# Gate logits of five chunks in four column quarters, and the gather of token rows moved ahead of the old output rows

## What is computed

```python
logits = x @ w_gate
noise_scale = np.log1p(np.exp(x @ w_noise))
noisy_logits = logits + noise_scale * noise
top2 = np.argpartition(-noisy_logits, 2, axis=1)[:, :2]
...
h = np.maximum(x[mask] @ w1[e], 0.0)
out[mask] += top2_w[mask, k, None] * (h @ w2[e])
```

## Time and profile before

| | us |
|---|---|
| median of 3 runs | 1023.05 |
| lowest, highest | 1022.73, 1024.32 |
| the profiled execution | 1022.97 |
| its span, first to last instruction | 1021.1 |

### The profile page before, as it was taken

How to read it: one execution, slowest core, us unless ns; L and a number is a source line. 1 busy time by engine, 2 the same in 40 slices (tenths; PEclk the granted TensorE clock), 3 DMA queues, 4 the chain that set the end, 5 groups by cost and what they waited for, 6 DMA issues and landing times.

```text
span 1021.1 us, 22022 instructions
## 1 busy us (share of the span) xinstructions
PE 1005.7 (98%) x5982; PEld 871.4 (85%) x5983; DVE 396.3 (39%) x784; ACT 430.6 (42%) x736; POOL 208.3 (20%) x198
## 2 busy tenths in 40 slices
PE   9999999999999999999999999999998999999996
PEld 7889999999999999999888888888887888888885
DVE  3565632432532423425553222242366354222221
ACT  3337754544555455557532222242354453222221
POOL 4540000020010200200332222222322232322222
PEclk9999999999999999999999999999999999999999
DMA  8753450000000000052316222243277342211111
GB/s 272 253 170 125 147 190 1 1 32 0 0 31 0 0 31 0 10 207 90 117 33 223 68 62 64 66 137 132 88 243 256 121 156 73 82 52 52 52 48 45
DMA packets 47078, 95.27 MB, mean 93 GB/s; under 512 B 19245, under 2 KB 24749, under 8 KB 42928
## 3 DMA queue, kind: packets, MB, share of 16 engines
q1 hardware_dynamic: 24240, 66.26, 19.2%
q0 software_dynamic: 10992, 27.84, 8.6%
q10 hardware_dynamic: 11808, 0.68, 0.8%
HBM read 78.98 MB, written 20.37 MB: 97 GB/s over the span
## 4 chain that ended last, share of the span: by engine, by line
PE 92%; DMA 3%; issue 2%; POOL 1%; ACTq 1%; DVE 0%; ACT 0%; SPq 0%; DVEq 0%; POOLq 0%
PE bank L701 27%; PE bank L703 26%; PE bank L702 26%; PE bank L833 3%; PE bank L780 2%; PE bank L652 2%; PE bank L626 2%; PE bank L756 1%; DMA xg<-x_rows,meta_x 1%; PE bank L645 1%; PE bank L612 1%; PE bank L665 1%; DMA out<-ysb,meta_y 1%; PE bank L750 1%; DMA lists<-rec,slot 0%
## 5 line engine op out<-in xcount | busy, mean ns | idle before, releaser
L701 PE MATMUL bank<-ew,hT_hi 128*128 (+1 forms) x328 | 131.9, 402 | 2.6 <-DVE hT_lo L1432 2.6
L701 PE MATMUL bank<-ew,xgT_hi 128*128 (+1 forms) x328 | 131.9, 402 | 0.7 <-issue 0.7
L701 PE MATMUL bank<-xs_hi,mw 128*128 (+1 forms) x384 | 130.0, 338 | 0.0
L703 PE MATMUL bank<-xs_hi,mw 128*128 (+1 forms) x384 | 129.6, 337 | 0.0
L702 PE MATMUL bank<-xs_lo,mw 128*128 (+1 forms) x384 | 129.0, 336 | 0.0
L703 PE MATMUL bank<-ew,xgT_lo 128*128 (+1 forms) x328 | 128.5, 392 | 0.0
L703 PE MATMUL bank<-ew,hT_lo 128*128 (+1 forms) x328 | 128.4, 391 | 0.0
L702 PE MATMUL bank<-ew,hT_hi 128*128 (+1 forms) x328 | 127.8, 390 | 0.0
L702 PE MATMUL bank<-ew,xgT_hi 128*128 (+1 forms) x328 | 127.6, 389 | 0.0
L520 POOL DMA_INDIRECT lists<-rec,slot x36 | 35.8, 994 | 389.5 <-DVE slot L1336 380.3
L701 PE MATMUL bank<-mw,g_hi 128*128 128x512 f32 x288 | 115.1, 399 | 0.0
(11 more groups left out here) (185 smaller groups left out, 1664.1 us busy)
## 6 DMA issues: line engine op xcount, KB each, us to landing
raw<-w_ex SPq DMA_DIRECT2D x32, 1024.0 KB
stage<-w_ff SPq DMA_DIRECT2D x16, 512.0 KB, 3.4
out<-blank SPq DMA_DIRECT2D x3, 1536.0 KB, 11.4
x_rows<-x2sb SPq DMA_DIRECT2D x6, 768.0 KB, 3.9
kbuf<-kN SPq DMA_DIRECT2D x16, 256.0 KB, 3.2
vbuf<-vN SPq DMA_DIRECT2D x16, 256.0 KB, 4.7
qbuf<-qT SPq DMA_DIRECT2D x15, 256.0 KB, 3.9
xg<-x_rows,meta_x POOLq DMA_INDIRECT x43
```

Source lines behind the costliest of these rows:

```text
L701: pe.matmul(o, a_hi, b_hi, start=first, stop=False)
L703: return pe.matmul(o, a_lo, b_hi, start=False, stop=last)
```

## The change

The gate of the five chunks: the three tiles' transposes come at steps 2, 3 and 4 of PE, and ACT copies them at the head of its steps 4, 5 and 6 into one transposed buffer of 384 tokens, for which the memory of `xs_hi` (for the last of the five, of `xs_lo`) is used, since that chunk's input is no longer needed. At step 5, four products with `wg` as the stationary operand (32 columns, 16 of them zeros) and 384 moving columns are formed, each block k of the width in column quarter k of the array, and so in partitions 32k to 32k+31 of bank 7. ACT copies the bank to `lgT` at the head of its step 7. At step 6, PE forms for each tile one product with `lgT` as the stationary operand and a matrix of zeros and ones (in `small`) that adds up the four quarters and turns the logits back. One copy by DVE at step 8 takes all 48 columns. PE's loop over four chunks becomes a loop of two passes with two chunks each. In the last chunk, steps below 10 use the ordinary activation buffer.

The experts: in POOL's step, the gather of tile g+3 comes ahead of the old rows of tile g. In ACT's step, the list of tile g+4 is asked for first, after a wait for the gather of tile g+2, which read the same buffer of `meta_x`.

```diff
+    small[:, 8:24] = i[:, None] % 32 == np.arange(16)
...
+        x2T_in, _ = place("x2T_in", [P, 2, KT, TOK], F32, R_T)
+        x2T_late, _ = place("x2T_late", [P, KT, TOK], F32, R_T + 2 * KT * TOK * 4)
...
-        x2T, R_C = place("x2T", [P, KT, P], F32, a)
+        lgT, R_C = place("lgT", [P, 512], F32, a)
...
-        wg, a = place("wg", [P, KT, 16], F32, a)
+        wg, a = place("wg", [P, KT, 32], F32, a)
...
             def step(i, s, last):
-                old_rows(s, i + 1, (i + s) * 16)
                 if not last:
                     gather_x(1 - s, i + s + 2, 2 * i + s + 2)
+                old_rows(s, i + 1, (i + s) * 16)
                 send_rows(s, 2 * i + s + 1)
...
-                pe.wait_ge(gate_kept, c * TJ + j)
+                else:
+                    pe.wait_ge(x2T_kept, c * TJ + j)
...
-            def gate_logits(c, j):
-                pe.wait_ge(x2T_kept, c * TJ + j + 1)
+            def gate_products(c, par):
+
+                pe.wait_ge(x2T_kept, c * TJ + TJ)
                 for k in range(KT):
-                    last = pe.matmul(gate_ps[:, 0:16], x2T[:, k, :], wg[:, k, :], start=(k == 0), stop=(k == KT - 1))
-                last.then_inc(gate_made, 1)
+                    last = pe.matmul(gate_ps[32 * k:32 * k + 32, 0:TOK], wg[:, k, :], (x2T_late if par is None else x2T_in[:, par])[:, k, :],
+                                     start=True, stop=True, tile_position=(0, 32 * k), skip_group_check=True)
+                last.then_inc(lgT_made, 1)
+
+            def gate_logits(c):
+
+                pe.wait_ge(lgT_kept, c + 1)
+                for j in range(TJ):
+                    last = pe.matmul(gate_ps[:, 16 * j:16 * j + 16], lgT[:, j * P:(j + 1) * P], small[:, 8:24],
+                                     start=True, stop=True)
+                last.then_inc(gate_made, TJ)
...
-            def gate_part(c, f):
-                if f in (2, 4, 6):
-                    gate_transpose(c, (f - 2) // 2)
-                elif f in (3, 5, 7):
-                    gate_logits(c, (f - 3) // 2)
+            def gate_part(c, f, par):
+                if f in (2, 3, 4):
+                    gate_transpose(c, f - 2)
+                elif f == 5:
+                    gate_products(c, par)
+                elif f == 6:
+                    gate_logits(c)
...
-            with pe.Fori(1, NCH - 1) as c:
-                ff_chunk(c, True, True)
-            ff_chunk(NCH - 1, True, False)
+            with pe.Fori(0, (NCH - 2) // 2) as i:
+                for u in range(2):
+                    ff_chunk(2 * i + u + 1, True, True, u)
+            ff_chunk(NCH - 1, True, False, None)
...
-                late = isinstance(c, int) and c == LAST
+                late = isinstance(c, int) and c == LAST and f >= LATE
...
+            def keep_products(c):
+                act.wait_ge(lgT_made, c + 1)
+                nc.scalar.activation(lgT[:, 0:TOK], gate_ps[:, 0:TOK], ACT.Copy).then_inc(lgT_kept, 1)
...
             def gate_part(c, f):
-                if f in (3, 5, 7):
-                    keep_x2T(c, (f - 3) // 2)
+                if f in (4, 5, 6):
+                    keep_x2T(c, f - 4)
+                elif f == 7:
+                    keep_products(c)
...
                 g = 2 * i + s
+                alone(act, got_x[s], i * 16 + 32)
+                load_meta(act, meta_x, s, g + 4, ld_mx[s])
                 split_hidden(g)
                 split_weights(g + 1, 0)
                 split_tile(g + 2, s)
-
-                load_meta(act, meta_x, s, g + 4, ld_mx[s])
                 next_tile(i, s)
...
-                if f in (4, 6, 8):
-                    keep_logits(c, (f - 4) // 2)
+                if f == 8:
+                    keep_logits(c)
```

More of the change, by code:

```diff
@@ L236, in build @@
         LAST = NCH - 1
+        LATE = 10
         bk = [bank(f"bank{i}") for i in range(4)]
@@ L285, in build @@
         x2T_made, x2T_kept, gate_made, gate_kept = (sem(n) for n in ("x2T_made", "x2T_kept", "gate_made", "gate_kept"))
+        lgT_made, lgT_kept = sem("lgT_made"), sem("lgT_kept")
         gate_exp, gate_log = sem("gate_exp"), sem("gate_log")
@@ L318, in as32, with x2T @@
             return ap.bitcast(F32)
+        def x2T(c):
+            if isinstance(c, int):
+                return x2T_late
+            return x2T_in[:, bass.ds(c % 2, 1), :, :].rearrange("p o k n -> p (o k) n")
         def q_of(t):
@@ L781, in tile_transpose, with ff_chunk @@
                 last.then_inc(xgT_made, 1)
-            def ff_chunk(c, gate, more):
+            def ff_chunk(c, gate, more, par=0):
                 for f in range(FT1):
@@ L791, in ff_chunk @@
                     if gate:
-                        gate_part(c - 1, f)
+                        gate_part(c - 1, f, par)
                     ff_out(c, f)
@@ L870, in last_gate_logits @@
                     for k in range(KT):
-                        last = pe.matmul(gate_ps[:, 16 * j:16 * j + 16], x2T_end[:, j, k, :], wg[:, k, :],
+                        last = pe.matmul(gate_ps[:, 16 * j:16 * j + 16], x2T_end[:, j, k, :], wg[:, k, 0:16],
                                          start=(k == 0), stop=(k == KT - 1))
@@ L1004, in keep_x2T @@
                 act.wait_ge(x2T_made, c * TJ + j + 1)
-                act.wait_ge(gate_made, c * TJ + j)
-                nc.scalar.activation(x2T[:, :, :], gate_ps[:, :].rearrange("p (k n) -> p k n", k=KT), ACT.Copy
+                nc.scalar.activation(x2T(c)[:, :, j * P:(j + 1) * P],
+                                     gate_ps[:, :].rearrange("p (k n) -> p k n", k=KT), ACT.Copy
                                      ).then_inc(x2T_kept, 1)
+            def keep_products(c):
+                act.wait_ge(lgT_made, c + 1)
+                nc.scalar.activation(lgT[:, 0:TOK], gate_ps[:, 0:TOK], ACT.Copy).then_inc(lgT_kept, 1)
             def gate_noise(c):
@@ L1242, in soft @@
                 n, t = c * FT1 + f, act_t[:, f % 2, :]
-                if isinstance(c, int) and c == LAST:
+                if isinstance(c, int) and c == LAST and f >= LATE:
                     t = late_t[:, f % 2, :]
@@ L1258, in keep_x2, with keep_logits @@
                     dve.tensor_copy(x2sb[:, j, :], acc_ps[j]).then_inc(x2_kept_v, 1)
-            def keep_logits(c, j):
-                dve.wait_ge(gate_made, c * TJ + j + 1)
+            def keep_logits(c):
+                dve.wait_ge(gate_made, c * TJ + TJ)
                 at_least(dve, gate_step, c * GATE_STEPS)
-                dve.tensor_copy(lg[:, j, :], gate_ps[:, 0:16]).then_inc(gate_kept, 1)
+                dve.tensor_copy(lg[:, :, :], gate_ps[:, 0:16 * TJ].rearrange("p (j n) -> p j n", j=TJ)
+                                ).then_inc(gate_kept, TJ)
             def chained(c, done, ins):
@@ L1607 @@
             moe_w_out.reshape(FT1, P, D)], axis=2)),
-        "w_gn": pack(np.concatenate([moe2_w_gate, moe2_w_noise], axis=1)),
+        "w_gn": pack(np.concatenate([moe2_w_gate, moe2_w_noise, np.zeros((D, 16), np.float32)], axis=1)),
         "noise": pack(moe2_noise.reshape(TILES, P, E).transpose(1, 0, 2)),
```

## The result

The changed kernel took 1016.93 us (median of 5 runs, 1015.1 to 1017.39) beside 1024.32 us for the one before in the same comparison: a ratio of 0.9926, 95% interval [0.9912, 0.994]. Two more comparisons of the same two kernels gave 0.9901 [0.988, 0.9922] and 0.9912 [0.9896, 0.9928]. The forecast was 1015.0 us, range 1013.5 to 1018.7. As a saving it was 8.0 us; the three comparisons, ratio times the time of before, have 7.6, 10.2 and 9.0. The profiled execution took 1015.1 us (span 1013.3), 7.9 less than the one of before.

A forecast was written before the change was run, and what follows sets the result against it. PE, busy 98% of the span, was taken as the bound, so time could come only from fewer passes or stalls: 1022.97 - 5.0 (gate) - 3.0 (expert loop) = 1014.97, so 1015.0 us, range 1013.5 to 1018.7.

The forecast's parts named there:

- Part 1: Gate of the five chunks: new products and logits take 1.67 us a chunk against 2.67, saving 5.0 us over five.
- products step: Gate, PE's step 5: eight passes of 384 columns in four column quarters add 1.0 us a chunk.
- logits: Gate, PE's step 6: three products 16 columns wide, six passes of 0.11 us, add 0.67 us a chunk.
- The factor for four at once: Gate products: four column quarters side by side run 3.0 times faster than in a row, as the attention's quadrants did.
- Part 2: Expert loop: the new orders of POOL and ACT remove two PE stalls, saving 3.0 us; ends 3.0 and nothing.
- The second stall: Expert loop: PE waits 1.50 us for gathered rows; with the gather issued first, they land before PE wants them.
- the first: Expert loop: PE waits 1.10 us for `hT_lo`, 1.35 with the refill; asking for the list earlier all but closes it.
- the 1.1 us leaves this chain: ACT's queue, expert loop: the list request moves to the step's head, so `hT_lo` is ready about 1.1 us sooner.
- Rival 1: Gate products: quarters overlap less; two at a time 1017.6 us (chance 0.10), one at a time 1024.3 (0.03).
- Rival 2: Expert loop: stalls only move, to `hT_lo` at the following tile; half or none saved, 1016.5 to 1018.0 us; chance 0.18.
- Rival 3: POOL's DMA queue: old rows behind the gather come late, PE loses 1.3 us nine times, 1030 us; chance 0.07.
- the added wait at ACT's head: Expert loop: ACT's wait for the gather of tile g+2 costs nothing, as POOL's new order issues that gather a step earlier.

The follow-up runs named there:

- the orders alone: Kernel before with POOL's and ACT's new orders in the expert loop and nothing of the gate change: 1020.30 us, ratio 0.9945.
- the two kernels that make it true: Changed kernel with a chunk's gate products on two column quarters instead of four, 1019.97 us, and on one, 1026.71 us.
- one copy more: Changed kernel with an extra 256 KB copy, result unused, behind each gather and ahead of the old rows: 1018.43 us, ratio 0.9957.

## Why the prediction was right, and where it was off

The mechanisms were those forecast: fewer passes of PE in the dense block, and two stalls of the loop gone or nearly so. That the sum came out close owes something to luck, as the terms show. Of the 1.9 us between 1015.0 and the measured 1016.93, 1.3 is the kernel before, at 1024.32 in the comparison and 1022.97 in the profile that the sum started from; 0.6 is the saving.

**Part 1** was 1.0 us a chunk and 5.0 in all; it is 1.06 a chunk (71.42 to 70.36 between rank products) and 5.71. The terms: products step 1.0 forecast, 0.97 measured; logits 0.67 and 0.65. The upper bound for eight passes in a row, 2.66, was measured as 2.70. The factor for four at once, taken from the quadrants as 3.0, is 2.70 / 0.78 = 3.5; the 0.1 for going back to the full array was about double (0.19 of the 0.97 lies outside the 0.78, 0.09 of it ahead of the group). The two errors cancel, by luck. The Trainium skill's page "TensorE: Matmul & The Clock Gate", section Measured speedup vs the span model, has 2.38 times for three column tiles; here two gave 1.9 and four 3.5, nearer to the ideal count. The 0.4 us over 1.06 x 5 is a term that I did not have: a wait of 0.20 us at the dense block's end (before at 497.25, first token rows' transposes), with its refill (the first passes after a wait start further apart), which the kernel with the orders alone keeps and all with the gate part lose. Why it goes was not tried.

**Part 2** was 3.0 us by the step lengths of one profile. The loop is 2.55 shorter in the profile of the result, 3.1 and 4.1 in the two later ones of the same kernel (454.85 and 453.84 us), and the comparison of medians gives 3.4. The 1.0 us between the last two is not stalls but the length of the ordinary step, 12.29 against 12.25 us. The second stall went as worked out. Of the first, forecast to all but close, 0.58 us is left (line 804 at 770.51, its successor at 771.44, against 0.35 without a wait). The step that was off is "the 1.1 us leaves this chain": the relu comes 0.78 us sooner behind `xgT_hi`, but the weights' first piece only 0.67 (3.70 us behind it, where it was 4.37, 764.32 to 768.69); ahead of that piece ACT then stands idle for 2.12 us, and its queue is in register loads. Whether these hold the last 0.33 us was not tried.

**Rival 1** (the quarters overlap less) is refuted by the two kernels that make it true: 1020.0 and 1026.7 us, where the rival had 1017.6 and 1024.3. **Rival 2** (the stalls only move) holds for 0 to 0.6 us: in the three profiles of the changed kernel the loop's stalls are 0.33, none and 0.18. **Rival 3** (old rows late) is refuted for the change itself: DVE waits for them less than before. The reason stands in the rows: they go out no later behind the write than they did. With one copy more it comes up in some runs.

What I under-rated is the added wait at ACT's head. It was costed at nothing, with the gather's landing as its cover, and the cover does hold, as POOL's new order makes it hold. Its price without the cover was not worked out; it is 9 us (1.0024 against 0.9936, which is from another comparison, for the same kernel with ACT's old order).

## What to carry to other kernels

When an edit adds a wait at the head of an in-order queue, work out its price without its cover as well, and look for the other part of the edit that provides the cover: here, on top of the gate part, POOL's order alone took 2.7 us off the loop (458.82 to 456.08), and ACT's alone cost 9. Small products side by side in column quarters came close to dividing their time by the number of quarters (2.70 us to 1.42 and 0.78), so it can pay to reshape a narrow product into that form even at the price of a second small product that adds up the quarters: here 0.97 + 0.65 us in place of 2.67, and a loss on one quarter. And an engine's long wait, here 53 us of ACT, says nothing before it is known who waits for that engine.

## What was not expected of the hardware

A stall of PE can cost more than its length: in the windows above, the clock drops to 0.50 of full speed behind stalls of PE, for 3.4 to 6.8 us. The length of the last stall does not decide it: 2.40 and 2.46 us had a drop behind them, the 2.71 us of the gate part alone had none. The clock also drops where PE was busy throughout. The kernel with the orders alone, two windows, columns as above:

```profile
500.00:505.00 5.00, 5.00 (x33) 4.33 (x31) 2.52 (x4) 4.12 (x7) 2.97 (x3) 1.00 0.64 141
505.00:510.00 5.00, 5.00 (x29) 4.45 (x29) 2.62 (x13) 2.79 (x5) 0.00 (x0) 0.72 0.22 73
```

This is where the gate of the last chunk is made, of many small passes; three of the fourteen profiles of this study show such a drop of 3.4 us there (1.7 us lost), and the others, those of before and after among them, do not. What decides it is open.

The gather's 256 KB lands in 3.4 us in the median of the changed kernel (over the gathers whose landing the profile shows, 4.8 at most), and took 8.16 in one place of the kernel with ACT's order alone, while weights were loading; 2.37 of it is POOL's own issue, which takes 1.02 in the changed kernel. That kernel's DMA queues from 750 to 762 us (packets, MB, share; q1, by its size, carries the weights, and the software queue q0 POOL's transfers):

```profile
q1 hardware_dynamic: 423, 3.10, 74.2%
q0 software_dynamic: 220, 0.52, 11.4%
```

The Trainium skill's page "DMA: Bandwidth & Descriptors", section Queues, rings and completion order, says that each DMA engine takes turns between the queues that have work, a packet at a time. By that the gather's rows should not wait for a whole weights piece; the trace has no more than the totals above and the 8.16 us, and does not settle it.
